# Operands moved in 48-row parts, buffers at multiples of 64 bytes, and the next pair's first right side between a dense stage's last down products

## What is computed

```python
# 1: recurrence, 4 batches x 8 heads, 768 steps, state 40 x 40 per head
for t in range(S):
    y[:, :, t] = einsum('bhd,bhde->bhe', rt, state)
    Sa = einsum('bhde,bhe->bhd', state, at)
    state_decay = state * wt[:, :, None, :] - einsum('bhd,bhe->bhde', Sa, bt)
    state = state_decay + einsum('bhd,bhe->bhde', vt, kt)
# 2: first dense stage, 3072 tokens, 320 -> 2048 -> 320
h = x @ w_in
x = (h - tanh(h)) @ w_out
# 3: four experts, 320 -> 1024 -> 320, p the normalised probabilities
for e in range(4):
    out += p[:, e:e + 1] * (maximum(x @ w1[e], 0) @ w2[e])
```

## Time and profile before

| | |
|---|---|
| median of 3 runs | 1630.55 us (1629.51 to 1633.9) |
| the profiled execution: its own time | 1631.27 us |
| its span in the profile | 1629.6 us |
| mean granted TensorE clock | 0.965 of full speed |
| busy: TensorE, VectorE, ScalarE, GpSimd | 1476.6, 835.4, 397.8, 365.1 us |
| DMA: moved, share of the 16 engines | 112.93 MB, 25% over the span |

### The profile page before, as it was taken

How to read it: one execution, slowest core, us unless ns; L and a number is a source line. 1 busy time by engine, 2 the same in 40 slices (tenths; PEclk the granted TensorE clock), 3 DMA queues, 4 the chain that set the end, 5 groups by cost and what they waited for, 6 DMA issues and landing times.

```text
span 1629.6 us, 37702 instructions
## 1 busy us (share of the span) xinstructions
PE 1476.6 (91%) x15888; PEld 1286.3 (79%) x15888; DVE 835.4 (51%) x1460; ACT 397.8 (24%) x814; POOL 365.1 (22%) x310
## 2 busy tenths in 40 slices
PE   2287687999999999999969999999999999999998
PEld 1266565977877887887858888989989898898887
DVE  7958855967867877765212233333333333332333
ACT  1022233333333333333323222111111111111111
POOL 4121253323323323221234300102020202020000
PEclk9987787999999999999989999999999999999999
DMA  7544585147127326112030220101010101000011
GB/s 180 159 116 124 157 213 148 31 115 195 48 78 198 82 61 176 48 42 58 9 87 18 85 69 1 36 0 36 0 36 0 35 0 35 0 0 0 0 48 48
DMA packets 89417, 112.93 MB, mean 69 GB/s; under 512 B 10952, under 2 KB 67400, under 8 KB 89288
## 3 DMA queue, kind: packets, MB, share of 16 engines
q1 hardware_dynamic: 89288, 111.05, 25.1%
HBM read 78.73 MB, written 32.28 MB: 68 GB/s over the span
## 4 chain that ended last, share of the span: by engine, by line
PE 79%; issue 9%; DVE 4%; POOLq 3%; POOL 3%; DMA 1%; ACT 1%; SPq 0%; DVEq 0%
PE banks L1522 22%; PE banks L1532 21%; PE banks L875 11%; PE banks L884 10%; PE banks L643 2%; POOLq L1299 2%; PE banks L758 1%; PE banks L706 1%; DVE nvmak L1179 1%; PE banks L736 1%; PE banks L723 1%; PE banks L715 1%; PE banks L762 1%; PE banks L616 1%; POOL wo L1321 1%
## 5 line engine op out<-in xcount | busy, mean ns | idle before, releaser
L1522 PE MATMUL banks<-x2t,u 128*128 (+1 forms) x1536 | 380.6, 394 | 0.0
L1532 PE MATMUL banks<-u,hid 128*128 128x320 f32 x2304 | 362.9, 309 | 0.0
L1532 PEld LDWEIGHTS banks<-u,hid 128*128 128x128 f32 x2304 | 350.7, 188 | 13.4 <-issue 0.9
L1626 DVE SCALAR_TENSOR_TENSOR hid<-banks,hid 128x512 fp32r<-128x512 f32 x192 | 132.9, 692 | 408.9 <-ACT hid L1612 408.9
L1522 PEld LDWEIGHTS banks<-x2t,u 128*128 128x128 f32 x1536 | 282.1, 188 | 56.5
L1612 ACT ACTIVATE hid<-banks 128x512 fp32r<-128x512 f32 x192 | 115.0, 599 | 569.1 <-PE banks L1522 569.1
L875 PE MATMUL banks<-xt,wi 128*128 128x512 f32 x768 | 200.1, 404 | 22.2 <-issue 13.3
L884 PE MATMUL banks<-wo,hid 128*128 128x320 f32 x1152 | 183.9, 309 | 5.7 <-POOL hid L1337 5.7
L884 PEld LDWEIGHTS banks<-wo,hid 128*128 128x128 f32 x1152 | 175.4, 188 | 14.2 <-POOL hid L1337 6.4
L875 PEld LDWEIGHTS banks<-xt,wi 128*128 128x128 f32 x768 | 143.8, 193 | 51.0 <-issue 14.8
L1337 POOL TENSOR_TENSOR hid<-shared,hid 128x512 fp32r<-128x512 f32 x96 | 123.7, 1288 | 225.2 <-ACT hid L1036 224.9
(11 more groups left out here) (117 smaller groups left out, 1570.8 us busy)
## 6 DMA issues: line engine op xcount, KB each, us to landing
scaled_operands<-made SPq DMA_DIRECT2D x41, 416.8 KB
made<-kbaw SPq DMA_DIRECT2D x41, 312.0 KB
kb<-scaled_operands SPq DMA_DIRECT2D x24, 416.0 KB
raw<-w SPq DMA_DIRECT2D x8, 640.0 KB, 5.8
lam<-scaled_operands SPq DMA_DIRECT2D x24, 209.6 KB
at<-scaled_operands SPq DMA_DIRECT2D x24, 208.0 KB
raw<-w SPq DMA_DIRECT2D x8, 512.0 KB, 4.0
rt<-rvt SPq DMA_DIRECT2D x96, 40.0 KB
```

Of the source, the lines that this page charges most:

```text
L1522: mm = pe.matmul(self.p_up[f][:], self.u1[:, par, w, f * 128:(f + 1) * 128], self.xt[:, bass.ds(n, 1), x, :].rearrange("p o t -> p (o t)") ...
L1532: mm = pe.matmul(self.p_dn[t][:, 0:D], self.hid[:, f, h, t * 128:(t + 1) * 128], self.u2[:, par, w, f, :], start=(f == 0 and i == 0), stop ...
L1626: dve.scalar_tensor_tensor(out=ex.hid[:, f, 1, :], in0=ex.p_up[f][:], scalar=0.0, in1=ex.hid[:, f, 0, :].bitcast(F32), op0=ALU.max, op1=AL ...
```

## The change

Loads, stores and reloads of a unit's operands are issued in two parts of rows, 56 or 48 rows and then 48: `row_parts(filled)` gives rows 0 to 55 and 56 to 103 where the buffer has not been filled yet (first loads into a slot, the stores of units 0 to 3, the reloads of pairs 0 and 1), and rows 0 to 47 and 56 to 103 afterwards; rows 48 to 55 are filling and stay. The load's a goes with the upper part in one DMA, so a load has three DMAs as before; stores, `kb`, `at` and `lam` have two instead of one. The semaphore counts follow. Buffers start at multiples of 64 bytes instead of 32, and a slot of `made` is padded from 5128 to 5184 bytes. In the dense stage down 12 moves behind up 15, and where a pair follows, its first right side (j = 0, b = 0) moves from the pair's start to between down 13 and down 14, and VectorE's mask of it ahead of its copies of the result banks.

```diff
--- before.py
+++ after.py
@@ -48,7 +48,9 @@
+LINE = 64
...
+ROWS = 48
@@ -164,9 +166,9 @@
     def sb(name, shape, dt=F32):
-        return outer.enter_context(nc.sbuf_tensor(name, shape, dt))
-
-    made = sb("made", [128, MADES, MADE])
+        return outer.enter_context(nc.sbuf_tensor(name, shape, dt, align_bytes=LINE))
+
+    made = sb("made", [128, MADES, -(-MADE // 16) * 16])
@@ -222,9 +224,14 @@
         to, a = raw_of(i), WW + OP_A
-        eng.dma_start(to[0:PR, 0:a], kbaw[i, :, 0:a]).then_inc(raw_op_in[slot(i)], 16)
-        eng.dma_start(to[0:HALF, a:a + 2 * C], kbaw[i, 0:HALF, a:a + 2 * C]).then_inc(raw_op_in[slot(i)], 16)
-        eng.dma_start(to[HALF:PR, a:a + 2 * C], kbaw[i, HALF:PR, a + 2 * C:a + 4 * C]).then_inc(raw_op_in[slot(i)], 16)
+        top, bottom = row_parts(before(i) is None)
+        eng.dma_start(to[top, 0:a + 2 * C], kbaw[i, top, 0:a + 2 * C]).then_inc(raw_op_in[slot(i)], 16)
+        eng.dma_start(to[bottom, 0:a], kbaw[i, bottom, 0:a]).then_inc(raw_op_in[slot(i)], 16)
+        eng.dma_start(to[bottom, a:a + 2 * C], kbaw[i, bottom, a + 2 * C:a + 4 * C]).then_inc(raw_op_in[slot(i)], 16)
+
+    def row_parts(filled):
+
+        return slice(0, PR - ROWS if filled else ROWS), slice(PR - ROWS, PR)
@@ -365,18 +372,19 @@
         def store_operands(i):
             sp.wait_ge(scaled, 2 * (i + 1))
-            sp.dma_start(scratch[i, :, :], raw_of(i)[0:PR, WW:MADE]).then_inc(op_stored[slot(i)], 16)
+            for part in row_parts(i < 4):
+                sp.dma_start(scratch[i, part, :], raw_of(i)[part, WW:MADE]).then_inc(op_stored[slot(i)], 16)
@@ -385,8 +393,9 @@
-            sp.dma_start(kb[:, p % 2, :, :, :, :].rearrange("p j a q t -> p j (a q t)"), both[:, :, 0:OP_A])\
-                .then_inc(kb_in[p % 2], 16)
+            for part in row_parts(p < 2):
+                sp.dma_start(kb[part, p % 2, :, :, :, :].rearrange("p j a q t -> p j (a q t)"), both[part, :, 0:OP_A])\
+                    .then_inc(kb_in[p % 2], 16)
...
@@ -606,8 +617,8 @@
                     pe.wait_ge(vn_in[p % 2], 16 * (p // 2 + 1))
-                    if p % PPC == 0 and p >= 2 * PPC:
-                        pe.wait_ge(up_saved, NF1 * (p // PPC - 1))
+                if p % PPC == 0 and p >= 2 * PPC:
+                    pe.wait_ge(up_saved, NF1 * (p // PPC - 1) - 1 + j)
                 pe.wait_ge(sc_saved[j], p + 1)
@@ -803,7 +814,8 @@
             more = p + 1 < NP
-            right_sides(p, 0, 0)
+            if not after_mlp:
+                right_sides(p, 0, 0)
             right_sides(p, 1, 0)
@@ -903,7 +915,9 @@
-                if f >= 2:
+                if f == NF1 - 1:
+                    down(c, f - 3)
+                if f >= 2 and f != NF1 - 2:
                     down(c, f - 2)
@@ -913,6 +927,8 @@
+            if last is not None and last + 1 < NP:
+                right_sides(last + 1, 0, 0)
             down(c, NF1 - 2)
             down(c, NF1 - 1)
@@ -1213,7 +1229,10 @@
-            sides(0)
+            if p and drained(p - 1):
+                save_right_side(p, 1, 0)
+            else:
+                sides(0)
@@ -1278,6 +1297,8 @@
+            if last is not None and last + 1 < NP:
+                save_right_side(last + 1, 0, 0)
             dve.wait_ge(dn_full, NF1 * (c + 1))
```

More of the change, by code:

```diff
@@ L189, in recurrence_and_first_mlp @@
     own = sb("own", [128, GH])
-    sb("between", [128, (ex.dense_at - -(-nc.sbuf_base // 32) * 32) // 4])
+    sb("between", [128, (ex.dense_at - -(-nc.sbuf_base // LINE) * LINE) // 4])
     assert nc.sbuf_base == ex.dense_at, (nc.sbuf_base, ex.dense_at)
@@ L210, in raw_of @@
         if t < MADES:
-            return made[:, t, :]
+            return made[:, t, 0:MADE]
         return (spare[:, t - MADES, :] if t < RING else shared[:, t - RING, :])[:, 0:MADE]
@@ L367, in load_raw @@
             if j is not None:
-                sp.wait_ge(op_stored[slot(j)], 16 * uses(j))
+                sp.wait_ge(op_stored[slot(j)], 32 * uses(j))
                 sp.wait_ge(lt_full, j + 1)
@@ L396, in load_a @@
                     sp.wait_ge(sma_full[j], NB * (p - 1))
-            a = at[:, p % 2, :, :, :].rearrange("p j q t -> p j (q t)")
-            sp.dma_start(a, both[:, :, OP_A:OP_LAM]).then_inc(at_in[p % 2], 16)
+            for part in row_parts(p < 2):
+                sp.dma_start(at[part, p % 2, :, :, :].rearrange("p j q t -> p j (q t)"), both[part, :, OP_A:OP_LAM])\
+                    .then_inc(at_in[p % 2], 16)
         def load_decays(p):
@@ L405, in load_decays @@
                 sp.wait_ge(state_ready, p - 1)
-            sp.dma_start(lam[:, p % 2, :, :, :].rearrange("p j q t -> p j (q t)"), both[:, :, OP_LAM:OPW])\
-                .then_inc(lam_in[p % 2], 16)
+            for part in row_parts(p < 2):
+                sp.dma_start(lam[part, p % 2, :, :, :].rearrange("p j q t -> p j (q t)"), both[part, :, OP_LAM:OPW])\
+                    .then_inc(lam_in[p % 2], 16)
         def turned_input(p, which):
@@ L462, in raw_piece @@
                 last = LAST_RAW[piece_slot(i)]
-                sp.wait_ge(op_stored[slot(last)], 16 * uses(last))
+                sp.wait_ge(op_stored[slot(last)], 32 * uses(last))
                 sp.wait_ge(lt_full, last + 1)
@@ L742, in scores @@
             if j == 0:
-                pe.wait_ge(kb_in[p % 2], 16 * (p // 2 + 1))
-                pe.wait_ge(at_in[p % 2], 16 * (p // 2 + 1))
+                pe.wait_ge(kb_in[p % 2], 32 * (p // 2 + 1))
+                pe.wait_ge(at_in[p % 2], 32 * (p // 2 + 1))
                 pe.wait_ge(r_in[p % 3], 64 * (p // 3 + 1))
@@ L951, in save_turned_answers @@
             if p == 0:
-                act.wait_ge(op_stored[RING + 1], 16)
+                act.wait_ge(op_stored[RING + 1], 32)
             act.activation(ut[:, :, :, :].rearrange("p j q t -> p (j q) t"),
@@ L1159, in mask_ur @@
             if p == 0:
-                dve.wait_ge(op_stored[RING], 16)
+                dve.wait_ge(op_stored[RING], 32)
             dve.tensor_tensor(out=nu[:, :, :, :, :].rearrange("p s j q t -> p s (j q) t"),
@@ L1185, in save_result @@
             dve.wait_ge(y_full, p + 1)
-            dve.wait_ge(lam_in[p % 2], 16 * (p // 2 + 1))
+            dve.wait_ge(lam_in[p % 2], 32 * (p // 2 + 1))
             if p:
@@ L1303, in decay_state @@
             pool.wait_ge(st_read, p + 1)
-            pool.wait_ge(lam_in[p % 2], 16 * (p // 2 + 1))
+            pool.wait_ge(lam_in[p % 2], 32 * (p // 2 + 1))
             both = st[:, g:g + 2, :, :].rearrange("p j q e -> p (j q) e")
@@ L1375, in __init__ @@
         self.probs, self.w1, self.w2, self.out = probs, w1, w2, out
-        place = [-(-nc.sbuf_base // 32) * 32]
-        self.dense_at = (nc.sbuf_usable_end - DENSE_WORDS * 4) // 32 * 32
+        place = [-(-nc.sbuf_base // LINE) * LINE]
+        self.dense_at = (nc.sbuf_usable_end - DENSE_WORDS * 4) // LINE * LINE
         def low(name, shape, dt=F32):
```

4 lines of the change are left out of this document (2 added, 2 removed).

## The result

| | before | after |
|---|---|---|
| median, us | 1632.22 (1629.51 to 1639.29, 4 runs) | 1606.99 (1605.92 to 1609.41, 4 runs) |
| ratio to before | | 0.9851, 95% interval 0.9824 to 0.9878 |
| profiled execution: time, span, mean granted clock | 1631.27, 1629.6, 0.965 | 1605.92, 1604.2, 0.975 |

In the kernel after, the lines stand 3 lines lower at the loads, 8 to 11 in the rest of SP's part, 11 or 12 in TensorE's, 16 in ScalarE's, 16 to 21 in VectorE's, 21 in GpSimd's and the experts'.

What follows compares the result with a forecast made beforehand. TensorE makes most of the chain of waits; before 280 us it idles while DMA engines are loaded. Terms 3.1 + 0.8 + 2.5 + 1.5 + 2.0 + 2.0 = 11.9 us off 1630.55 gave 1618.7 us, range 1611 to 1627.5.

Steps and rivals of the forecast that it cites:

- Padding and alignment: Buffer starts and padded slots of made: taken as zero, bounds from nothing to the whole of the waits for DMA landings.
- the four waits: Places priced for DMA landings: unit 15, the starts of pairs 5 and 6, and the start of the first dense stage.
- Unit 15: VectorE's and TensorE's wait for unit 15's load: a quarter less landing time, 2.5 us, bounds 0 to 3.7.
- rival B: TensorE's clock stays up after shorter idle times at three places, up to 2 us each: 1612.7 us; chance 0.15.
- Start: Issue of the first seven units' 21 loads before the first scan: 0, bounds -2.2 to +1.5 us.
- Pairs 5 and 6 and the first dense stage: Shorter waits for landings there: 1.5 us at pair 5, 2.0 at pair 6, 2.0 at the first dense stage.
- The 120 added DMAs: SP's extra issues, about 0.4 us each: no cost after 280 us while SP's lead lasts.
- The dense stages' ends: New order: 0.52 us earlier at six stage ends, 0.2 us at four seams to the next pair, 3.9 us.
- Rival C: Transfers are bound elsewhere than by the number of engines; only the new order gains: 1626.6 us; chance 0.20.
- part 2: The new order at the end of the dense stages, six stages and four seams, forecast at 3.9 us.
- 13 full engines: DMA share near 0.81 at 195 to 205 us read as 104 rows on 13 of 16 engines, three idle.
- Rival D: SP is held on added DMAs too, about seven at 1.5 us ahead of the landings: slower, 1638.7 us; chance 0.10.

Runs made afterwards that it cites:

- r13: The changed kernel, unchanged, run again in a later batch: 1605.12 us, ratio to before 0.9865.
- e1: The kernel before with the 48-row parts alone, buffers and order as before: 1615.89 us, ratio 0.9936.
- e4: The kernel before with the parts alone, but cut into rows 0 to 51 and 52 to 103: 1622.24 us, ratio 0.9965.
- e5: The kernel before with the 48-row parts alone, the first seven units still loaded in the old form: 1619.64 us, ratio 0.9927.
- e10: The changed kernel with parts of 52 and 52 rows: 1611.71 us, ratio to before 0.9903.
- e2: The kernel before with the 64-byte alignment and padded slots alone: 1625.02 us, ratio 0.9983.
- e3: The kernel before with the new order at the end of the dense stages alone: 1621.13 us, ratio 0.9952.
- e6: The kernel before with only the buffer x2t moved by 32 bytes, to a multiple of 64: 1624.24 us, ratio 0.9968.
- e9: The kernel before with only down 12 moved behind up 15, the right side left in place: 1624.46 us, ratio 0.9981.
- e8: The changed kernel with three units loaded ahead of the start's barrier and the other four behind it: 1604.36 us, ratio to before 0.9839.
- e12: The kernel before with unit 15's load issued ahead of the stores of units 11 to 13 in pair 1: 1622.24 us, ratio 0.9956.
- r14: The changed kernel with parts of 56 and 48 rows throughout, so all 104 rows move: 1608.35 us, ratio to before 0.9880.
- r15: The changed kernel with unit 15's load issued ahead of the stores of units 11 to 13: 1605.29 us, ratio to before 0.9857.
- e11: The changed kernel with three units loaded ahead of the barrier and unit 15's load ahead of the stores of units 11 to 13: 1600.82 us, ratio 0.9832.

## Why the prediction was wrong

The direction was right, and so were most of the mechanisms. The sum failed: one step that has a price was taken as nothing, and others were too small. Its range also was narrower than its own terms: their bounds added up make 1610 to 1632 us and not 1614 to 1624, and the measured 1607.0 lies below either. By its own steps, with the means of several traces where one does not decide:

- **Padding and alignment: forecast 0, measured 4.5 us.** This is the step that failed outright, "I take zero; its bounds are those of the four waits". The bounds left out that an address can change the pace of the engine that reads there. From 1000 us on TensorE works 624.8 of 629 us; there every ns of a matmul is on the path, and the 1536 up products each lost 2 to 3. It could have been asked from the profile: two kinds of matmul fill that stretch, and the buffer that one of them reads was to move. The answer could not: the same move of xt is worth nothing in the dense stages.
- **Unit 15: forecast 2.5 us, measured about 5.** The landing got 3.3 us faster (9.5 to 6.3), more than the quarter of it that was reckoned; and rival B's clock came on top here, 2.1 us from the answer to the state product. B was given 0.15 and priced at up to 2 us a place: the price was right, the chance was not. At 165 us the traces with parts stand a mean 7.3 us ahead of before's (six of them: after, r13, e1, e4, e5, e10), those without 1.0 (before with its 0, e2, e3, e6, e9); less 1.1 us, the mean of the six for the earlier start, that is about 5.
- **Start: forecast 0, measured 1.2 us** earlier at the first scan, inside the bounds of -2.2 to +1.5. A unit's three DMAs take 1.32 us for 1.45. How much of it reaches the end is open (e5), and e8 shows 5.3 us of such a gain swallowed.
- **Pairs 5 and 6 and the first dense stage: forecast 5.5 us, measured 1.8.** From 165 us to the first dense stage the six traces with parts gain a mean 2.0 us on before's, the five without 0.2. ScalarE's waits at the first piece and at the tokens did not shorten but grew: all that is ahead of them moved up by some 9 us, while the pieces of weights that they wait for come in their old form. Read so, it was the error of pricing a wait at its present length when the work ahead of it moves too; no run varies it by itself.
- **The 120 added DMAs: forecast 0 after 280 us; a cost is not to be seen.** The opposite: from the first dense stage to the experts the traces with parts and the old order gain 2.9 us (mean of e1, e4, e5) on those with neither (before, e2, e6, e12, and e9 less its 2.5). 2.1 of it lie in the pairs behind the second dense stage. "No wait of TensorE names a load" there; which wait gets shorter was not found, and with three traces against five it stays open.
- **The dense stages' ends: forecast 3.9 us, measured 3.9 at the ends and some 2 behind them.** The 3.9 are 6 x 0.42 + 4 x 0.34 instead of 6 x 0.52 + 4 x 0.2, so that they meet is in part luck. The wait that takes the place of the old one, for down 12's buffer, is there: ScalarE's copy starts 0.1 us behind down 12's end, and the low half follows. The rest, 2.3 us over the 3.9 in the seven traces with parts and the new order against e1, e4 and e5 (1.1 in e3, without parts), no term had; most of it is at pair 12, where the prediction looked for nothing ("Behind the new position no engine queues") and TensorE's idle time of 1.1 us went away.

Start 1.1, unit 15 5.1, the waits up to the first dense stage 1.8, the parts behind it 2.9, the order 3.9 and 2.3, and the experts 4.5 make 21.6 us; each term but the order's 3.9 and the experts' rests on means of few traces, good to about 1 us. The two single traces are 25.4 apart, because before's lies 2.9 us behind the mean of its like (1.0 at 165 us, 0.2 up to the first dense stage, 1.7 behind it) and after's 0.9 ahead of its own.

The signs that the prediction named came true at three places: idle time at the stages' ends 0.39 (about 0.3), VectorE's wait at unit 15 3.35 (below 4), and the first dense stage at 263.59 (about 266). The fourth, a DMA share over 0.81 with more GB/s, was there in the one trace and tells nothing, since e9 with whole transfers shows 0.88 and 0.89. Rival C, transfers bound elsewhere with nothing left but part 2, is out: e1 alone gives 10 us, and 48 rows beat 52 at unit 15. The Trainium skill's port rule (SBUF — State Buffer, Door 1: The DMA port swizzle) was cited for C; by it 48-row parts would bring nothing, and unit 15's 6.3 us for 9.5 do not agree. The Trainium skill's rule on the number of engines (DMA: Bandwidth & Descriptors, Why a DMA increments its semaphore by 16 and not by 1) is not settled by these runs: by it e9's 104 rows use 13 of 16 engines, 0.81, and its share of 0.88 and 0.89 is above that, as is before's own 0.87 at 98 us, though transfers of other shapes run in these windows too. r14, by it on 14 and 16 engines, takes 7.7 us at unit 15, no less than e10's 7.1 on 13. So the step from 0.81 to "13 full engines" is not shown; what is shown is that 48 rows help. Rival D is out too: SP is held 0.48 us at unit 15's load, not 1.4, and of its DMAs up to 280 us 10 are held over 1.2 us, 17 before.

## What to carry to other kernels

In a stretch where one engine is busy throughout, ask of every buffer that is moved who reads it there: an address can cost or give a fraction of a percent of that whole stretch, with no wait to point at it, and whether it does is to be measured: here one buffer gave it and its like, moved by the same 32 bytes, did not. A wait that is taken from an engine whose clock falls at it is worth more than its length, and its price turns on whether the clock still falls at the idle time that is left; a wait further down is not worth its present length, since all ahead of it moves too. A change of order can take away idle time at a place that it does not name; the same idle time, looked up in all traces, tells which edit it goes with. And one trace is one execution: here four traces of the same instructions differed by 7 us at the same row, so small terms are to be read from medians, or from differences between two rows that lie close together.

## What the runs showed of the hardware that was not expected

- The up products of the experts, whose moving operand is x2t (128 x 512 fp32r columns), take 392 ns each with x2t at a multiple of 64 bytes and 394 with it 32 bytes past one, in all 17 traces, and by the move of that one buffer (e6). It is no general rule: in the dense stages the same move of xt gave 395.0 for 395.1 ns (e2 and before). The down products kept 309 ns whether hid2, their stationary side, was moved or not.
- Behind one answer TensorE worked at a granted clock of 0.50 in the ten traces in which it had idled 0.91 to 4.58 us ahead of it, and at 1.00 in four in which it had idled 0.54 us, 0.45 or not at all (after, r13, e12, r15). The three others (e8, e11, r14) were still in an earlier stretch at 0.50.
- The same instructions up to 165 us took 7 us more in one trace than in another; from 85 us on, the clock was at its lower level for 51.2 us in the slower (e6) and 17.1 in the faster (e9).
- 104 rows in two DMAs land sooner than in one: 9.5 us from issue to use with whole transfers around it (five traces), 7.6 with 52 and 52 or 56 and 48 rows (three), 6.3 with 48 and 48, which leave 8 rows out (five).
